# Attention, routed experts and a feed-forward in one program: the router split by batch and placed inside attention, the first expert job run while the last batch is routed

## The reference

```
# attention: 8 heads of 64, window of 128 keys back, linear bias
scores = where(mask, scale * q @ k.T + bias, -1e9); x = softmax(scores) @ v
# routed experts: 8 experts, 512 -> 1024 -> 512
do = x @ w_skip > 0;  logits = x[do] @ w_gate
e_idx = argmax(logits);  gate_w = softmax(logits)[e_idx]
y[e_idx == e] = gate_w * (relu(x @ w1[e]) @ w2[e]);  out[do] = x + y
# feed-forward: 512 -> 2048 -> 512
h = x @ w_in;  out = (h * tanh(softplus(h))) @ w_out
```

## Time and profile before

| | |
|---|---|
| median of 3 runs | 751.3 us (751.11 to 751.73) |
| profiled execution | 752.2 us, its span 750.4 us |
| mean granted clock of PE | 0.989 |
| busy: PE, DVE, ACT, POOL | 97%, 68%, 49%, 15% |
| attention | up to about 145 us |
| router and first gather | about 145 to 170 us |
| ten expert jobs | about 170 to 330 us |
| feed-forward | from about 330 us |

### The profile page before, as it was taken

One profiled execution on the slowest core, in us unless ns is written; L12 is line 12 of the kernel. 1 busy time (PEld: TensorE's weight loads), 2 busy tenths in 40 slices (PEclk: granted clock), 3 DMA queues, 4 the chain that ended last, 5 costly groups with the idle time before them and its releaser, 6 DMA issues.

```text
span 750.4 us, 13457 instructions
## 1 busy us (share of the span) xinstructions
PE 731.6 (97%) x4452; PEld 566.8 (76%) x4452; DVE 509.6 (68%) x1270; ACT 365.0 (49%) x879; POOL 109.1 (15%) x254
## 2 busy tenths in 40 slices
PE   7999999989999999998999999999999999999997
PEld 5888888783333333357898899998988998999986
DVE  4777777651111111669998888888788888888885
ACT  5888888401011011736565554555465555545444
POOL 5566666111120110100000000000000000000000
PEclk8999999979999999999999999999999999999999
DMA  8788897317784570031010101101010101001001
GB/s 277 268 257 272 280 287 237 91 36 274 267 315 170 226 290 17 21 108 41 1 43 1 43 0 43 43 1 33 12 42 0 42 0 42 0 0 43 1 0 43
DMA packets 53244, 78.23 MB, mean 104 GB/s; under 512 B 24739, under 2 KB 26403, under 8 KB 53152
## 3 DMA queue, kind: packets, MB, share of 16 engines
q1 hardware_dynamic: 51136, 72.02, 28.8%
q0 software_dynamic: 1600, 4.85, 1.7%
q10 hardware_dynamic: 432, 0.41, 0.2%
HBM read 65.53 MB, written 12.56 MB: 104 GB/s over the span
## 4 chain that ended last, share of the span: by engine, by line
PE 89%; DVE 6%; issue 3%; ACT 2%; POOL 0%; DVEq 0%; SPq 0%; ACTq 0%; POOLq 0%
PE ps_y L1458 16%; PE ps_ht L1440 13%; PE ps_xt L1440 12%; PE ps_y L1139 9%; PE ps_h L1121 9%; PE ps_h L1458 8%; PE ps_out_t L588 5%; PE ps_scores L561 4%; PE ps_probs_t L572 4%; PE ps_x L600 3%; DVE h_sb L1031 1%; PE ps_y L90 1%; PE ps_ht L1128 1%; PE ps_h L1426 1%; PE ps_x L607 1%
## 5 line engine op out<-in xcount | busy, mean ns | idle before, releaser
L1329 ACT ACTIVATE u_sb<-u_sb 128x384 f32<-128x384 f32 x96 | 50.6, 527 | 104.6 <-DVE u_sb L1377 104.6
L1333 ACT ACTIVATE r_sb<-n_sb,all_consts 128x384 f32<-128x384 f32 x96 | 59.3, 617 | 85.3 <-DVE n_sb L1393 85.3
L397 ACT ACTIVATE probs<-probs,neg_max 128x256 f32<-128x256 f32 (+2 forms) x160 | 72.6, 455 | 17.1 <-DVE neg_max L455 16.8
L1458 PE MATMUL ps_y<-ffn_hi,g_lo 128*128 128x512 f32 x192 | 76.3, 397 | 0.0
L1458 PE MATMUL ps_y<-ffn_hi,g_hi 128*128 128x512 f32 x192 | 76.1, 396 | 0.0
L1458 PE MATMUL ps_y<-ffn_lo,g_hi 128*128 128x512 f32 x192 | 75.7, 394 | 0.0
L1405 DVE SCALAR_TENSOR_TENSOR u_sb<-n_sb,r_sb 128x384 f32<-128x384 f32 x96 | 53.6, 559 | 19.2 <-ACT r_sb L1335 19.2
L1440 PE MATMUL ps_ht<-xt_hi,ffn_lo 128*128 128x384 f32 x192 | 65.8, 343 | 0.2 <-DVE xt_lo L1368 0.2
L1440 PE MATMUL ps_xt<-xt_hi,ffn_lo 128*128 128x384 f32 x192 | 65.7, 342 | 0.0
L1440 PE MATMUL ps_ht<-xt_lo,ffn_hi 128*128 128x384 f32 x192 | 65.0, 339 | 0.0
L1440 PE MATMUL ps_xt<-xt_lo,ffn_hi 128*128 128x384 f32 x192 | 65.0, 339 | 0.0
(11 more groups left out here) (177 smaller groups left out, 1615.5 us busy)
## 6 DMA issues: line engine op xcount, KB each, us to landing
w_sb<-in_w SPq DMA_DIRECT2D x8, 2048.0 KB, 11.4
ffn_raw<-in_w_ffn SPq DMA_DIRECT2D x16, 512.0 KB, 4.9
experts_even<-in_w SPq DMA_DIRECT2D x16, 512.0 KB, 5.7
experts_even<-in_w SPq DMA_DIRECT2D x4, 2048.0 KB, 11.8
q_raw<-in_qT SPq DMA_DIRECT2D x15, 288.0 KB, 3.9
k_raw<-in_kT SPq DMA_DIRECT2D x15, 288.0 KB, 5.0
v_sb<-in_v SPq DMA_DIRECT2D x16, 256.0 KB, 2.6
tokens<-x_out SPq DMA_DIRECT2D x64, 64.0 KB, 3.9
```

Of the source, the lines that this page charges most:

```text
L397: nc.scalar.activation(probs[0:n, r, h, 0:w], probs[0:n, r, h, 0:w], ACT.Exp, bias=neg_max[0:n, r, h:h + 1], scale=-1.0, accum_out=sums[0: ...
L1329: nc.scalar.activation(u_sb[:, t.r], u_sb[:, t.r], ACT.Exp).then_inc(u_ready, 1)
L1333: nc.scalar.activation(r_sb[:, t.r], n_sb[:, t.f % NB], ACT.Ln, bias=cst["two"]).then_inc(ln_ready, 1)
L1458: m = nc.tensor.matmul(ps_o[i][:, :], a[:, t.r, P * i:P * i + P], ffn[b][:, at:at + D], start=(t.f == 0 and n == 0), stop=(t.f == FT - 1 a ...
```

## The change

1. A class `Router` holds the router's tensors and steps for one batch each. Its tensors lie where four of the feed-forward pieces (10 to 13, `MID`) used to be loaded in attention; those are now loaded after the first gathers.
2. In attention, `routing(r)` gives for each round a batch and a step. The three early batches start at rounds 14, 24 and 34; step 0 sums logits, 1 chooses, 2 ranks and weighs, 3 finds rows, 4 marks the first job and makes one-hot rows, 5 adds the list. PE's products for it stand ahead of the scores of a round's second tile. POOL multiplies and numbers, ACT exponentiates and spreads, SP stores the weights of each batch.
3. The first job of pair 0 takes the first 64 tokens of experts 0 and 1 among the first three batches. Its rows are gathered by POOL before attention's last four rounds of gate copies. If an early batch set were short, `shift` pads the ranks behind it; here it isn't.
4. After attention PE starts with that job. The last batch's rank products stand between the halves of its hidden layer, the table's products between the halves of its output; then comes the transpose of the second job and the reading of the counts. ACT clips the first hidden layer. All `keep_warm` calls go.
5. Each pair has its own number of unconditional jobs, `SURE` = 2, 1, 1, 2. The second job is gathered from its own column of the table.
6. The first layer of pair 1 is loaded at attention's end, over the dead q, k and bias buffers, one load ahead of the last pair's stores and one behind them; its second layer after the second gather.

The diff, cut to what the steps touch:

```diff
+    def choose(self, dve, b):
+        dve.wait_ge(self.cst["logits_added"], b + 1)
+        then(v.tensor_reduce(top, lg, AX_X, ALU.max))
+        v.tensor_tensor(self.shifted[:, t], lg, over_top, ALU.subtract).then_inc(self.shifted_ready, 1)
...
+        v.tensor_tensor_scan(self.upto[:, b].rearrange("p e t -> p (e t)"), self.same_expert,
...
+    def number_tokens(self, pool, b):
...
+        pool.wait_ge(self.row_found, b + 1)
+        pool.wait_ge(self.side_ready, b + 1)
...
+    def first_job(self, dve, b):
...
+        dve.wait_ge(self.placed, b + 1)
...
+    def rank_products(self, pe, b, ps_rank, ps_early=None, ps_count=None):
...
+        pe.wait_ge(self.chosen_ready, b + 1)
...
+        t_.matmul(ps_rank, self.not_before, hot, start=True, stop=False)
+        m = t_.matmul(ps_rank, self.ones, upto, start=False, stop=(b == 0))
...
+    SINCE = HP * QT // 2 + LAG_X + 1
...
+            if n >= 6 and n % HP == 2:
+                router.store_weights(sp, n // HP - 1, dram)
...
+        w1 = list(pair_weights(dram, cst["w_sb"], 1))[0:2]
+        sp.wait_ge(router.first_in[0], 16)
+        sp.wait_ge(scores_ready, GROUPS)
+        sp.dma_start(*w1[0]).then_inc(cst["w1_loaded"][1], 16)
         for i in range(QT):
             store(PAIRS - 1, i)
+        sp.wait_ge(max_ready, 2 * GROUPS)
+        sp.dma_start(*w1[1]).then_inc(cst["w1_loaded"][1], 16)
...
-            if r % (HP * QT // 2) == 6 and r > HP * QT // 2:
-                add_logits(r // (HP * QT // 2) - 1)
+            b, step = routing(r)
...
+            if step == 0:
+                add_logits(b)
+            if step == 1:
+                router.choose(dve, b)
+            if step == 2:
+                router.read_rank(dve, b, ps_rank, ps_early)
+                router.find_side(dve, b)
+            if step == 4:
+                router.first_job(dve, b)
+                router.make_rows(dve, b)
+            if step == 5:
+                router.add_first(dve, b, ps_first, ps_behind)
...
+            if step == 2:
+                router.weigh(dve, b)
+            if step == 3:
+                router.place_tokens(dve, b)
+                router.mark_pairs(dve, b)
...
-        keep_warm(nc, ps_out_t, cst, 10)
...
+        copy_first(0)
+        router.exps(act, B - 1)
+        relu_first(0)
+        relu_first(1)
+        router.spread(act, B - 1)
         act.wait_ge(jobs_ready, 1)
         totals = [jobs_of(act, p) for p in range(PH)]
-        copy_first(0)
...
+        def first_of_all():
+            hidden(0, 0, 0)
+            router.rank_products(pe, B - 1, ps_rank, ps_count=ps_count)
+            hidden(0, 0, 1)
+            transpose_h(0, 0, 0)
+            transpose_h(0, 0, 1)
+            output(0, 0, 0, 0)
+            make_table()
+            output(0, 0, 0, 1)
+            pe.wait_ge(table_ready, 1)
+            transpose_x(0, 1, 1)
+
...
+        transpose_first(0)
+        first_of_all()
         pe.wait_ge(jobs_ready, 1)
         totals = [jobs_of(pe, p) for p in range(PH)]
-        transpose_first(0)
```

More of the change, by code:

```diff
@@ L132, in sb, with attention @@
+def attention(nc, ctx, buffers, block, dram, ffn, cst, router, x_in):
     def sb(name, shape, dt=F32):
@@ L440, in _ @@
                         round_k(t.pair + 1)
+            b, step = routing(r)
+            if step == 1:
+                router.exps(act, b)
+            if step == 3:
+                router.spread(act, b)
     @block.vector
@@ L738, in experts @@
     y_scattered = by_phase("y_scattered")
[L740 to L745 removed]
+    ident = cst["ident"]
     half = F1 // 2
@@ L1000, in _ @@
[L1000 to L1006 removed]
+        v, then = nc.vector, functools.partial(router.then, dve)
+        v.memset(y_sb[:, D:ROW], 0.0)
@@ new lines, in _ @@
+        router.choose(dve, B - 1)
+        router.weigh(dve, B - 1)
+        router.find_side(dve, B - 1)
+        router.mark_pairs(dve, B - 1)
+        router.read_rank(dve, B - 1, ps_rank)
+        v.tensor_scalar(count_i, ps_count, float(W - 1), None, ALU.add)
+        dve.wait_ge(router.rank_ready, B)
+        then(v.tensor_copy(router.rank_i, router.rank[:, router.tiles(B - 1)]))
+        v.tensor_scalar(router.row_i, router.rank_i, W - 1, None, ALU.bitwise_and)
+        then(v.tensor_scalar(count_i, count_i, LOG_W, None, ALU.logical_shift_right))
@@ L1015, in _ @@
-        then(v.tensor_reduce(job1, work, AX_X, ALU.add))
-        then(v.tensor_tensor(job1, job1, rank, ALU.add))
-        by_job = [P, TT, JOBS]
-        then(v.tensor_tensor(in_job, cst["job1"].unsqueeze(1).broadcast_to(by_job),
-                             job1.unsqueeze(2).broadcast_to(by_job), ALU.is_equal))
-        v.tensor_tensor(what[:], in_job, number.unsqueeze(2).broadcast_to(by_job), ALU.mult)
-        for i in range(0, TT, LT):
-            v.tensor_tensor(at_row[:, i:i + LT], tab["rows"].unsqueeze(1).broadcast_to([P, LT, P]),
-                            row[:, i:i + LT].unsqueeze(2).broadcast_to([P, LT, P]), ALU.is_equal
-                            ).then_inc(rows_ready, 1)
+        then(v.tensor_tensor(by_phase_work, router.pair_hot, first1.unsqueeze(1).broadcast_to([P, TT, PH]), ALU.mult))
@@ new lines, in _, with compare @@
+        then(v.tensor_reduce(job1, by_phase_work, AX_X, ALU.add))
+        dve.wait_ge(router.placed, B)
+        then(v.tensor_tensor(job1, job1, router.chunk, ALU.add))
+        by_job = [P, QT, JOBS]
+        def compare(b):
+            t = router.tiles(b)
+            v.tensor_tensor(in_job[:, t], cst["job1"].unsqueeze(1).broadcast_to(by_job),
+                            job1[:, t].unsqueeze(2).broadcast_to(by_job), ALU.is_equal).then_inc(compared, 1)
+        compare(0)
+        for b in range(B):
+            if b + 1 < B:
+                compare(b + 1)
+            if b == B - 1:
+                router.make_rows(dve, b)
+            t = router.tiles(b)
+            dve.wait_ge(compared, b + 1)
+            v.tensor_tensor(what[:, t], in_job[:, t], router.number[:, t].unsqueeze(2).broadcast_to(by_job), ALU.mult
+                            ).then_inc(what_ready, 1)
```

523 lines of the change are left out of this document (351 added, 172 removed).

## The result

| | before | after |
|---|---|---|
| median | 751.75 us (749.02 to 753.67, 20 runs) | 756.04 us (750.28 to 759.55, 20 runs) |
| ratio | | 1.005, 95% interval 1.003 to 1.0071 |
| profiled execution, span | 752.2, 750.4 us | 750.75, 748.7 us |
| mean granted clock | 0.989 | 0.993 |

A forecast was written before the change was run, and what follows sets the result against it. PE, 97% busy with 89% of the chain, was taken to bound the kernel; 752.2 + 7.2 (attention) - 14.35 (first two jobs) + 4.0 (clock) = 749.05 us profiled, 748.1 us as median, range 741 to 755.

The forecast's parts named there:

- the first two jobs: Behind attention: job 1's hidden layer starts at 172.7 instead of 187.05 us, a gain of 14.35 us before clock losses.
- Attention, the step that failed: Router work for three batches moved into attention costs 2.4 us a batch, 7.2 us in all; ends 1 and 12.
- PE's additional products: In attention: 9 to 10 more small products, 1.0 us a batch, mostly under rounds DVE sets; 0.3 us is left.
- DVE's work, 5.35 us a batch: In attention: the router's new DVE operations, from choosing to the list, take 5.35 us together in each early batch.
- Six rounds offer 6 x 0.70 = 4.2 us: In attention: DVE's spare 0.70 us a round over six rounds hides 4.2 us of a batch's router work.
- POOL, 0.6 us of DVE waiting: In attention: DVE waits twice a batch for POOL, busy splitting q and k; 0.6 us of waiting.
- The clock, 4 us lost: Around the second gather: PE's idle of 3.0 and 2.8 us brings ten us at half rate; 4 us lost, ends 0 and 5.
- rival 2: Clock falls while ACT reads its counts, slowing job 0's first output half and the table: 5.8 us more, 753.9; chance 20%.
- Register reads: Around the first two jobs: 0.7 us a read; ACT's cost 1.4 us, PE's four take 2.8 us before job 1.
- rival 4: At the first two jobs: register reads cost next to nothing as queues run ahead, 744.5 us; chance 7%.
- Rival 5: After attention: stores behind 4 MB of weights land late, second gather waits until 166 instead of 162.8, 751 us; chance 8%.
- Pair 1's start comes with the same shift: At pair 1's first product, before at 202.39 us: its start moves earlier by as much as job 1's.

The follow-up runs named there:

- e12: e9 with the token-counting scan's mask read from PSUM instead of SBUF in the early batches: 739.19 us, ratio 0.9835 to the kernel before.
- e4: Changed kernel with the row comparison split into five VectorE operations with one tensor input each: 753.55 us, ratio 1.0032 to the kernel before.
- e5: Changed kernel with VectorE instead of POOL doing the two small operations on rows and numbers in attention: 746.26 us, ratio 0.9936 to before.
- e6: Changed kernel with the row comparison in attention reading its row numbers from PSUM, POOL still numbering: 749.03 us, ratio 0.9971 to before.
- e7: Changed kernel with the edits of e5 and e6 both at once: 746.57 us, ratio 0.9946 to the kernel before.
- e1: The changed kernel unedited, run again for a second trace: 755.4 us, ratio 1.0044 to the kernel before.
- e2: Changed kernel with 8 keep-warm products ahead of job 0's output and 14 behind it: 754.65 us, ratio 1.0045 to the kernel before.
- e3: Changed kernel with PE's count reads before its second-gather wait and ACT's behind its copy of job 0's hidden layer: 751.74 us, ratio 1.0006 to before.
- e10: e9 with ten keep-warm products in the wait for the second gather: 744.59 us, ratio 0.9885 to the kernel before.
- e11: e9 with the marking of pairs for all batches moved from attention to the tail: 740.68 us, ratio 0.9843 to the kernel before.
- e8: e3 with four feed-forward pieces loaded behind pair 2's weights instead of ahead of pair 1's start: 746.04 us, ratio 0.9933 to before.
- e9: Changed kernel with the edits of e3, e5, e6 and e8 together, without keep-warm: 739.75 us, ratio 0.9835 to the kernel before.

## Why the prediction was wrong, step by step

**The clock in the profiled execution.** The sum was made for one execution, 749.05 us; its like, after's profile, is 750.75. The steps between: attention +4.3 (9.2 us at its end plus a start that was 2.3 us quicker, 11.5, against 7.2), the start -2.3 (before's half-rate stretch at 11 to 18 us is missing in this execution), the first two jobs with their clock -1.3 (27.6 + 2.75 of half rate in job 1's hidden layer, against 27.7 + 4), the transposes of pair 1's first job +0.7, the gap +1.1. That makes 751.55; the 0.8 us less lie behind pair 1's start and were not followed. That this execution comes within 1.7 us of the forecast is luck in part: attention's excess and the quicker start nearly cancel. The median is another matter, since a typical execution has more half-rate stretches.

**Attention, the step that failed.** 7.2 us were forecast, 2.4 a batch; 11.5 were measured at full clock (4.79, 4.22 and 2.50). Of the 4.79, PE's own busy time is 1.79 and its idle time 3.00. One term is shown to be wrong: the hold-up of DVE by POOL, which the sum had at nothing, with the wait for POOL beside it, which it had too short. A second is likely too small: PE's additional products, put at 0.3 us. Terms:
- DVE's work, 5.35 us a batch: measured 6.27 in ten rounds, but 2.30 of it are two hold-ups (1.06 the scan, 1.24 the comparison). Its own work was about 4, less than I had.
- "Six rounds offer 6 x 0.70 = 4.2 us": not shown wrong, and not shown right. In e12, without hold-ups, DVE has 4.96 us more work than before in the first ten rounds, and they are 3.09 longer. But of these 3.09, 2.28 are PE's busy time and only 0.81 its idle time. So between 1.9 us (if PE's products cost nothing) and 4.15 (if they cost their full length) of DVE's work were hidden. The second ten rounds have none of the one-time products; in them, before and e12:

```profile
86.54:119.23 32.69, 32.53 (x382) 28.17 (x380) 25.73 (x118) 27.42 (x99) 21.32 (x53) 1.00 0.89 274
```

```profile
90.25:125.69 35.44, 34.17 (x390) 29.35 (x388) 29.82 (x144) 27.90 (x101) 21.64 (x54) 1.00 0.76 218
```

Here DVE has 4.09 us more, PE is busy 1.64 and idle 1.11 longer. That DVE's new work does push the maxima behind it can be seen in ACT, whose exponentials wait for them: 17.1 us over the run before, 22.9 in e12, 28.4 in after:

```profile
L711 ACT ACTIVATE probs<-probs,neg_max 128x256 f32<-128x256 f32 (+2 forms) x160 | 72.6, 455 | 28.4 <-DVE neg_max L774 28.3
```

- POOL, 0.6 us of DVE waiting: 1.02. The place was right, the size short.
- PE's additional products, 0.3 left of 1.0: PE's busy time is 1.79 and 1.69 us longer in the two batches. PE was idle for 0.16 us in ten rounds before, so its new work finds room only where PE would wait for DVE; how much of it does the runs don't separate.
- The hold-up of DVE by POOL's two-input subtractions: not in the sum at all. Taking it and the wait for POOL out shortens ten rounds by 1.70 and 1.47 us (e12), and with the idle of PE go the clock falls inside attention. The comparison took 2.06 us with both inputs in SBUF and 0.82 with one in PSUM, and POOL's subtraction 1.84 instead of 1.40 where DVE had started first. By the Trainium skill, page "SBUF — State Buffer", section "Who interferes with whom", a DVE operation with two SBUF inputs contends with a GpSimd operation that reads SBUF, and whoever issues first has the port pair until it is done. The runs agree on both points. The same section says that some one-input forms, `tensor_scalar` among them, can take both pairs if their operands meet certain conditions, and then contend too, which would fit the 2.24 us of e4; no run here tests it.

**The clock, 4 us lost.** In the tail its size was right: in after, the half rate costs 1.8 us in job 0's output and 2.75 in job 1's hidden layer. Its first place was rival 2's, "one gap earlier": PE was idle 1.73 us and the clock was at half rate behind it, which the prediction itself named as a sign against it. But it lasted some 4 us, not the ten of the earlier trace rows, and so cost 1.8, not 5.8. In e5, e6 and e7, with the same code there, job 0's output runs at full rate (3.65 us). What no case had is a fall inside attention: ten rounds grow by 2.5 and 1.5 us in e1, by 1.1 and 1.5 in e2.

**The median.** The forecast put it 0.9 us below the profiled execution; it lies 5.3 above. The one further profile of the unedited kernel is e1's, which is the slowest of its executions, so what follows is the far end and not the middle. From after's profile to e1's, 748.7 to 759.0 us of span: 6.6 up to attention's end (160.82 against 154.24), of which 2.6 up to round 14, where e1 has half rate (16 to 20 us) and after's profile has not, and 2.5 and 1.5 in the two batches. Then job 1's hidden layer 2.5 quicker, the gap 2.62 instead of 1.06, a hidden layer behind it at half rate (8.62), and two stretches of the feed-forward at half rate, of which one window here:

```profile
350.00:354.00 4.00, 4.00 (x14) 3.41 (x14) 3.73 (x8) 2.40 (x6) 0.00 (x0) 0.57 0.02 4
```

After's own profile has 1.00 in it. These last stretches lie in code that the change did not touch. Why they come stays open: e3, e4, e6, e10 and e11 have one or two as well, before, after, e2, e5, e7, e8, e9 and e12 none.

**Right.** The first expert product 1.1 us after attention. Job 1 after 27.7 us (27.6, in e1 27.7). Register reads cost: rival 4 falls, since e3 takes 3.3 us out by moving them. A read is 0.4 to 0.56 us in these rows (ACT four in 1.7, PE four in 2.25 of which 1.65 lie behind ACT's copy), not 0.7: the place was right, the size by a quarter to two thirds too large. Rival 5 falls: the second gather was issued 0.9 us after its list was ready.

**Also off.** From DVE's table to the gathered rows 4.9 us (174.07 to 178.94), not 6.6: what made the first gather of before longer was not tested. "Pair 1's start comes with the same shift": it did not. I had costed the four moved pieces at nothing, by their landing times; the cost (1.1 to 2.7 us of gap, and a clock fall behind it in e1 and e3) was in none of my terms.

## What to carry to other kernels

Work moved under a full engine costs that engine too: PE had 0.16 us free in ten rounds, and its few small products for the router made its own busy time 1.6 to 1.8 us longer. The prediction watched DVE, which had 7 us free. Before work is moved beside another engine's, look which operations it will meet: a DVE operation with two SBUF inputs that meets a POOL subtraction can take several times its length, and one input in PSUM, or an earlier start, frees it. And a median can move by idle stretches of about two microseconds, through the clock: the edit of e5 shortens attention by 2.2 us in the profile and the run by 8. Compare several executions, not one profile of each.

## What the runs showed of the hardware that I had not expected

- A hold-up at a port does not show as a wait. It is inside the busy time of the operation: 2.06 us against 0.81, 1.30 against 0.24. The view that finds it is the spread of durations of one operation with one shape.
- Idle of PE of 1.83 to 1.86 us was followed by half rate in two profiled executions (e1, e2; 2.02 us in e4), for some 3.4 to 6.8 us, and by full rate in three others (after, e3, e8).
- PE stood 0.8 to 2.7 us at the start of pair 1 with all semaphores there, while weights and pieces filled the queues (after, e1 to e7); with the pieces (2 MB) later it was 0 to 0.64 us (e8 to e12). Where there is such a gap of 0.3 us or more, PE's first product comes 1.54 to 1.60 us behind the end of a transfer of instructions.
